# Moving the stores of six weight blocks, and where ScalarE prepares keys, queries and x, in an attention and two-FFN kernel

## The reference

```python
scores = scale * q @ k^T + minimum(-(cum[i] - cum[j]), 0), causal   # 8 heads of width 64
x   = softmax(scores) @ v                                            # heads side by side: 576 x 512
h   = relu(x @ w_in)                                                 # 512 -> 1024
x1  = (h * sigmoid(conv3(h, conv_w))) @ w_out                        # 1024 -> 512
u   = x1 + (x1^T @ U @ V)^T                                          # rank 32 over the positions
out = u + relu(u @ w_ch1) @ w_ch2                                    # 512 -> 2048 -> 512
```

## Time and profile before

| | us |
|---|---|
| median of 3 runs | 909.82 |
| lowest and highest run | 908.84, 910.62 |
| the profiled execution's own time | 910.62 |
| span of the profiled execution | 908.8 |
| PE busy | 861.6 (95%) |
| DVE busy | 468.5 (52%) |
| ACT busy | 372.5 (41%) |

### The profile page before, as it was taken

One profiled execution on the slowest core, in us unless ns is written; L12 is line 12 of the kernel. 1 busy time (PEld: TensorE's weight loads), 2 busy tenths in 40 slices (PEclk: granted clock), 3 DMA queues, 4 the chain that ended last, 5 costly groups with the idle time before them and its releaser, 6 DMA issues.

```text
span 908.8 us, 15655 instructions
## 1 busy us (share of the span) xinstructions
PE 861.6 (95%) x6184; PEld 809.2 (89%) x6184; DVE 468.5 (52%) x984; ACT 372.5 (41%) x709; POOL 50.6 (6%) x105
## 2 busy tenths in 40 slices
PE   4888898989999999999999999999999999999998
PEld 3666888879998999889998999988999999999998
DVE  6788694464445934555344871455323761442222
ACT  2777675554425634544332653444221431221110
POOL 3021000000000000000000000000000000000000
PEclk9999998989999999999999999999999999999999
DMA  7686945636663557336545454435444444274441
GB/s 162 164 228 157 305 141 189 222 73 199 214 209 104 188 167 259 127 106 212 180 152 177 129 172 145 134 100 184 146 145 169 141 174 150 94 240 182 150 175 53
DMA packets 64396, 150.36 MB, mean 165 GB/s; under 512 B 30026, under 2 KB 44362, under 8 KB 51780
## 3 DMA queue, kind: packets, MB, share of 16 engines
q1 hardware_dynamic: 61252, 144.50, 49.4%
q0 software_dynamic: 3072, 4.87, 2.1%
HBM read 119.15 MB, written 30.11 MB: 164 GB/s over the span
## 4 chain that ended last, share of the span: by engine, by line
PE 66%; DVE 13%; issue 10%; ACT 5%; DMA 4%; POOL 1%; SPq 1%; DVEq 0%; ACTq 0%; POOLq 0%
PE psum L1190 18%; PE psum L1192 18%; PE psum L1191 17%; PE psum L1169 5%; DVE work L958 2%; DVE psum L899 2%; PE psum L1116 2%; DVE work L961 2%; DMA few_scratch<-few 2%; PE psum L1148 2%; PE psum L1146 2%; DMA spread_out<-few_scratch 2%; DVE work L956 1%; ACT work L746 1%; DVE ybuf L973 1%
## 5 line engine op out<-in xcount | busy, mean ns | idle before, releaser
L1190 PE MATMUL psum<-r_hl,ring 128*128 128x288 f32 x512 | 153.6, 300 | 3.2 <-DVE r_hl L1001 1.7
L1190 PE MATMUL psum<-uu_hl,ring 128*128 128x288 f32 x512 | 153.2, 299 | 1.5 <-DVE r_hl L1001 1.5
L1192 PE MATMUL psum<-r_hl,ring 128*128 128x288 f32 x512 | 151.2, 295 | 0.0
L1191 PE MATMUL psum<-r_hl,ring 128*128 128x288 f32 x512 | 151.1, 295 | 0.0
L1192 PE MATMUL psum<-uu_hl,ring 128*128 128x288 f32 x512 | 151.0, 295 | 0.0
L1191 PE MATMUL psum<-uu_hl,ring 128*128 128x288 f32 x512 | 150.9, 295 | 0.0
L783 ACT ACTIVATE r_hl<-psum 128x288 fp32r<-128x288 f32 x128 | 52.5, 411 | 188.1 <-PE psum L1192 188.0
L1001 DVE SCALAR_TENSOR_TENSOR r_hl<-psum,r_hl 128x288 fp32r<-128x288 f32 x128 | 58.5, 458 | 134.7 <-ACT r_hl L783 134.6
L1169 PE MATMUL psum<-probs,va 128*65 128x320 f32 (+4 forms) x448 | 109.6, 364 | 6.5 <-ACT probs L694 6.3
L899 DVE CUSTOM_DVE_ANT_0 psum<-psum,key_late 128x512 f32<-128x512 f32 (+4 forms) x160 | 84.9, 564 | 57.1 <-PE psum L1116 56.8
L1190 PEld LDWEIGHTS psum<-r_hl,ring 128*128 128x128 f32 x512 | 96.6, 189 | 5.5 <-DVE u_acc L1013 2.7
(11 more groups left out here) (101 smaller groups left out, 1626.6 us busy)
## 6 DMA issues: line engine op xcount, KB each, us to landing
ring<-w_scratch SPq DMA_DIRECT2D x74, 1024.0 KB, 4.9
w_scratch<-ring SPq DMA_DIRECT2D x24, 1024.0 KB, 6.1
kq_raw<-in_kq_t SPq DMA_DIRECT2D x64, 288.0 KB, 5.0
stage<-in_w_ch SPq DMA_DIRECT2D x16, 512.0 KB, 4.7
spread_out<-few_scratch POOLq DMA_DIRECT2D x32, 144.0 KB, 3.2
out_t<-u_acc SPq DMA_DIRECT2D x16, 288.0 KB, 3.7
va<-in_v SPq DMA_DIRECT2D x32, 128.0 KB, 2.8
stage<-in_w_out SPq DMA_DIRECT2D x4, 512.0 KB, 6.5
```

Source lines behind the costliest of these rows:

```text
L1190: pe.matmul(o, hi, m_hi, start=start, stop=False)
L1191: pe.matmul(o, hi, m_lo, start=False, stop=False)
L1192: return pe.matmul(o, lo, m_hi, start=False, stop=stop)
```

## The change

1. `STORE_STEPS` goes. Each block made in image 0 is stored in image 0. For the first five, the store is issued in the step (h, 1) after the head that made it, ahead of the next `load_raw`, at h = 2, 3, 5, 6 and 7. The sixth is stored after the last step of image 0, ahead of image 1's first load of keys and queries.
2. On ACT, in images 1 to 3, `prepare_keys` moves from behind the FFN items of step g = 2 to ahead of them, and `prepare_queries` from behind those of g = 3 to ahead of them. DVE's low parts stay where they were.
3. x's high and low parts for images 1 to 3: pair 0 moves from (4, 0) to (3, 4), pair 1 from (6, 0) to (5, 4), pair 2 from the start of the next image to (7, 4), and for the last image from item 0 of `END` to (7, 4) too.
4. ACT's high part of u (`u_high`) for a `mix` item that is the last of its step moves from behind the next attention step to ahead of it.

```diff
-        STORE_STEPS = [(0, 4), (1, 0), (1, 1), (1, 2)]
-        END_INVERT, END_NORMALISE, END_SPLIT = 2, 5, {0: NPAIR - 2, 6: NPAIR - 1}
+        END_INVERT, END_NORMALISE, END_SPLIT = 2, 5, 6
-        X_SPLIT = [{(5, 0): 0, (7, 0): 1}, {(4, 0): 0, (6, 0): 1}]
-        X_SPLIT_LAST = [{}, {(0, 2): (NPAIR - 2,), (1, 0): (NPAIR - 1,)}, {(0, 0): (NPAIR - 2,), (0, 2): (NPAIR - 1,)}]
+        X_SPLIT = [{(5, 0): 0, (7, 0): 1}, {(3, 4): 0, (5, 4): 1, (7, 4): 2}]
+        X_SPLIT_LAST = [{}, {(0, 2): (NPAIR - 2,), (1, 0): (NPAIR - 1,)}, {(0, 2): (NPAIR - 1,)}]
@@ sync, attention_step
-                    if a == 1 and (h, g) in STORE_STEPS:
-                        store_block(MADE[len(EARLY) + STORE_STEPS.index((h, g))])
@@ sync, image 0
                     if g == 1 and h - 1 in WEIGHTS_HEADS[:-1]:
-                        nth = WEIGHTS_HEADS.index(h - 1)
-                        if nth < len(EARLY):
-                            store_block(MADE[nth])
-                        load_raw(nth + 2)
+                        store_block(MADE[WEIGHTS_HEADS.index(h - 1)])
+                        load_raw(WEIGHTS_HEADS.index(h - 1) + 2)
+                store_block(MADE[len(WEIGHTS_HEADS) - 1])
                 bodies(attention_step, ffn_step)
@@ scalar, attention_step
-                    if g == 3 and not a:
-                        prepare_keys(a, h + 2)
+                    if g == 3:
+                        if a == 0:
+                            prepare_keys(a, h + 2)
                         prepare_queries(a, h + 2)
...
-                def then(a, h, g):
-                    if g == 2:
+                    if g == 2 and a:
                         prepare_keys(a, h + 2)
-                    if g == 3:
-                        prepare_queries(a, h + 2)
@@ scalar, follow and ffn_step
-                    if kind == "mix" and half:
-                        u_high(b, i)
...
                         g_high(b, half)
+                    if kind == "mix" and half:
+                        u_high(b, i)
```

More of the change, by code:

```diff
@@ L838, in _ @@
                 act.wait_ge(s_hid, 1)
-                bodies(body_step, ffn_step, then)
+                bodies(body_step, ffn_step)
                 follow(PLAN[B - 1][-1][-1])
                 for x, item in enumerate(END):
-                    if x in END_SPLIT:
-                        x_high(B - 1, END_SPLIT[x])
+                    if x == END_SPLIT:
+                        x_high(B - 1, NPAIR - 1)
                     ffn_step(item)
@@ L1080, in _ @@
                         normalise_few(B - 1, NPAIR - 1)
-                    if x in END_SPLIT:
-                        x_low(B - 1, END_SPLIT[x])
+                    if x == END_SPLIT:
+                        x_low(B - 1, NPAIR - 1)
                     ffn_step(item)
```

## The result

| | before | after |
|---|---|---|
| median of 8 runs each, us | 909.36 | 914.81 |
| lowest and highest | 908.35, 910.62 | 912.23, 918.43 |
| the profiled execution's own time | 910.62 | 910.87 |
| its span | 908.8 | 909.1 |

The ratio is 1.0055, 95% interval 1.0034 to 1.0077: slower by 5.0 us (3.1 to 7.0). Two further sets of runs gave 1.0049 (1.0030 to 1.0068) and 1.0063 (1.0047 to 1.0079). Three executions, of 1188, 2128 and 4030 us, are set aside; two of them were the profiled ones of e3 and e5, so these two have no trace that can be read.

What follows compares the result with a forecast made beforehand. PE, busy 95% of the span, was taken as the bound, with idle time mainly in early stretches. Terms 2.2 + 0 + 0.3 + 0.1 - 0.8 + 1.1 = +2.9 us gave 912.7 us; 8-in-10 range 907.8 to 917.5.

Steps and rivals of the forecast that it cites:

- Spread and gathers land 2.6 and 3.0 us later: POOL's transfers issued at 81 to 83 us, slowed by the sixth store; inversion and PE's chain 2.2 us late.
- the upper bound: Stores' cost of up to 4.4 us, if head 7's new store also holds up the pair's small store near 76 us.
- Raw loads: 0, bounds 0 and 1: Head 6's raw load, behind a store, lands at 68.7 us, before ACT wants it at 69.39: 0 us.
- rival B: Stores hidden: POOL's transfers pass them, or DVE and PE have slack; +0.7 us, 910.5; chance 0.21.
- Changes 2 to 4: +0.7: Moves on ACT in images 1 to 3: 0.3 + 0.1 - 0.8 + 1.1 us.
- the first fall: Clock fall at 138 to 142 us, in PE's 2.88 us wait; copies ahead of y's high part cost 0.3 us.
- The wait of 0.72 us ahead of 129.94 us: PE's wait for exponentials, saved as ACT is free sooner; -0.8 us over the kernel, bounds 0 and -3.
- The evictions of (5, 4): Image 1: pair 1's x_high and one u_high ahead of the exponentials of 195.44 us; cost 1.1 us, bounds 0 and 1.4.
- rival A: Third clock fall, as PE's wait at 88 us grows to 2.6 us; 2.3 us more, 915.0; chance 0.15.
- the signs of being wrong: First x product at 96 us or sooner; changed number of clock falls; over 3 us gained or lost after 220 us.
- C: Faster: PE's waits before both clock falls shrink, the 2.88 us one under about 2, clock stays up; 907.1; chance 0.14.
- D: ACT's moves delay evictions in images 2 and 3 too, some 16 steps at 0.3 us, +4.8 us; 917.5; chance 0.08.

Runs made afterwards that it cites:

- e3: Kernel before with only the sixth store moved to the end of image 0: 909.11 us against 908.77, ratio 1.0004 (0.9978 to 1.0029).
- e5: Kernel after, unchanged, run again: 913.23 us against 908.40 for before; its profiled execution was set aside.
- e4: Kernel before with only the stores at heads 5, 6 and 7 moved into image 0: 911.61 us against 908.77, ratio 1.0019 (0.9999 to 1.0039).
- e7: Kernel before with only the store at head 7 moved into image 0: 911.37 us against 908.40, ratio 1.0044 (1.0029 to 1.0060).
- e1: Kernel before with change 1 alone, all six stores in image 0: 912.47 us against 908.77, ratio 1.0035 (1.0015 to 1.0055).
- e6: Kernel before with only the sixth store moved to 82 us, second set: 910.18 us against 908.40, ratio 1.0013 (0.9994 to 1.0033).
- e9: Kernel after, the four moved stores sending only their high half in image 0, low half in image 1: 911.44 us against 908.80, ratio 1.0030.
- e11: Kernel after, unchanged, run again with a second readable profile: 914.38 us against 908.80 for before.
- e8: Kernel before with only the stores at heads 5 and 6 moved into image 0: 909.10 us against 908.40, ratio 1.0016 (0.9996 to 1.0037).
- e2: Kernel after with the stores put back, so changes 2 to 4 alone: 909.46 us against 908.77 for before, ratio 0.9996 (0.9975 to 1.0018).
- e12: Kernel after with the stores put back, changes 2 to 4 alone, second set: 910.38 us against 908.80 for before, ratio 1.0017.
- e10: Kernel after with the store of head 7 and the sixth back in image 1: 912.71 us against 908.80 for before, ratio 1.0045.

## Why the prediction was right, and where its size was off

Forecast +2.9 us (912.7), measured +5.0 us (3.1 to 7.0).

*Spread and gathers land 2.6 and 3.0 us later.* They landed 2.1 and 3.4 us later. The inversion came 2.98 us late, where 2.2 was forecast, and PE's wait grew by 2.74 us. Right in place and nearly in size. Of the chain I took the gathers alone as the link that comes last. In the first profile DVE's multiplication, held by the spread, was 2.47 us late already (88.29 against 85.82), and the gather added 0.5 us; in e4 and e7 the spread alone held the inversion, in e1, e6, e9 and e11 the gather came last. And I gave the sixth store as the one that the small transfers meet; e4, e6 and e7 show that the store of head 7, six microseconds earlier, delays the spread, and alone costs 4.0 us (1.7 us together with those of heads 5 and 6, in e4), while the sixth costs 0.4 to 1.2 us alone. I had head 7's store only in the upper bound, and there by way of the pair's small store.

*Raw loads: 0, bounds 0 and 1.* The block of head 6, which I priced, made ACT wait 0.52 us; its load took 8.5 us to land, not 7.3. The block of head 7, which I did not price, made it wait 2.03 us, since its load took 9.6 us. I had taken one load behind one store; here the load of the head before landed at 68.8 us (60.30 + 8.5), when the next store had been issued at 67.93 us. A wait of 0.97 us of this kind in e8 left PE's wait near 88 us as it was.

*Packets take turns (rival B, +0.7).* The small transfers were slowed by 2.1 and 3.4 us, and rival B fell. The rule that the Trainium skill gives ("DMA: Bandwidth & Descriptors", section "Queues, rings and completion order") may hold as it stands, and no run here can show the order of the packets. But it does not make a 2 KB transfer free beside a store: 6.4 us against 3.0 here.

*Changes 2 to 4: +0.7.* Measured +0.6 (-0.4 in e2, +1.5 in e12). The pieces are there. PE's wait at the first fall is 3.25 us in after instead of 2.88, +0.37 for 0.3 forecast. The wait of 0.72 us ahead of 129.94 us is gone, as counted. The evictions of (5, 4) delay the exponentials so that PE waits 1.83 us at the values of the next step, where it did not wait before, while the wait of 1.20 us just ahead of it shrank to 0.83 us:

```profile
142.79 0.43 PE L1121 MATMUL psum<-ident_r,row_max 128*1 128x128 f32 x5 [3.25 <-DVE row_max L891]
...
195.92 0.40 PE L1253 MATMUL psum<-v,ybuf 96*128 96x288 f32 x1 [0.83 <-DVE work L983]
198.16 1.11 PE L1161 MATMUL psum<-probs,va 128*65 128x320 f32 x2 [1.83 <-ACT probs L689]
```

That nets +1.46 for the 1.1 forecast. DVE's wait for the keys, 13.7 us in the earlier trace rows, is no longer among the sixty longest, and that for the queries fell from 12 times and 15.5 us to 3 times and 11.3 us. Together that is more than half gone, and PE gained nothing by it, as forecast.

```profile
DVE qb L878 <- ACT qb L676: 11.3, 3, 7.2
```

*Clock, and what the sum lacked.* I left a third fall of the clock out of the sum, as rival A with a chance of 0.15. A changed number of falls stood among the signs of being wrong, and it changed. The +5.0 us measured is what rival A's sum gives, 2.9 + 2.3 = 5.2, and the forecast's +2.9 lies just under the measured interval; that the time is within the range of 907.8 to 917.5 owes something to the width of that range. All six profiles with a store at head 7, or half of one (after, e1, e4, e7, e9, e11), show a clock of 0.63 to 0.88 between 82 and 96 us. Before, e2, e6 and e8 show 1.00. Two profiles without that store, e10 and e12, show 0.76; in both the clock had already fallen once in image 0. Over all executions the mean clock fell from about 0.9925 to 0.988. In the three sets of before, an execution's time rises by 0.44 to 0.58 us for each 0.001 of clock lost, so 0.0045 less goes with 2.0 to 2.6 us. With the +2.9 of the sum that makes 4.9 to 5.5 us. This is a fit over executions and not an experiment on the clock; that the clock causes this part is argued, not shown.

Nor can head 7's store be given all of the lost clock. Against the before of the same chip, the mean fell by 0.0042 and 0.0057 in the two further sets of after (e11, e5), but by 0.0020 with change 1 alone (e1), 0.0015 with head 7's store alone (e7), 0.0008 and 0.0017 with changes 2 to 4 alone (e2, e12), and by 0.0057 in e10, where that store is in image 1. So the terms stand like this. The stores were forecast at 2.2 us and cost 3.2 alone; by the fit 0.9 to 1.2 us of that goes with the clock. Changes 2 to 4 were forecast at 0.7 and cost 0.6. The last 1.2 us of the 5.0 appears only where both are in the kernel, unless it is chance, and there more clock is lost than both lose alone (0.0028 to 0.0037 together). Why, stays open.

*Rivals C and D.* No fall of the clock vanished for good (C): the profiled execution of after has weaker falls at 140 and 200 us (0.81 and 0.86 for 0.62 and 0.72), and gives back 2.3 us by there. PE starts the `up` products 1.5 us late, having been 3.8 us late at its first x product. From the `up` products to the end it makes up 1.2 us more: in before the clock is still low there (0.59 us for the first of them, 0.38 in after). That is part of why its total was 0.3 us from before's while the median was 5 us away. C's condition did not come: the wait of 2.88 us, which had to fall under 2 us, grew to 3.25. D fell: PE's idle time after 220 us did not grow.

## What to carry to other kernels

A bulk store put into a stretch whose own transfers already keep the DMA engines 0.78 busy (the mean from 16 to 82 us in before) can cost time even if no engine waits for the store itself. Look for the small transfers that something does wait for, and price them by the landing times beside an earlier store, counting also a store issued five microseconds ahead of them (75.86 and 81.14 us in after) and not only the nearest. Where a PE wait grows toward one at which the clock fell before (here 2.88 us), put a fall of the clock into the sum. A single profiled execution can be the lucky one, so compare the mean clock over all of them.

## What was not expected

With the same program, executions differ in how often PE's clock falls: three and five times in the two profiles of after, three and five in those of e2 and e12, and two to six over all twelve. Between 50 and 54 us, in image 0, it fell in e10, e11 and e12 and in no other profile, though all these kernels run the same program up to there. PE waits of 2.64 to 3.37 us near 88 us came with a low clock in five profiles out of five, and those of 2.87 to 3.26 us near 140 us in all twelve; the wait of 1.55 us in e6 did not. The length of a wait does not decide alone: between 178 and 185 us all twelve have one of 1.45 to 1.50 us, and the clock fell near it in six (e2, e4, e7, e10, e11, e12) and not in the other six. The falls near 184 and near 200 us both stand in four of the six profiles with changes 2 to 4 (e2, e10, e11, e12) and in none of the six without them, where there is only one of the two.
